# Two-layer network behind attention: the state-row softmax turned in 32x32 blocks by VectorE in place of TensorE's transposes, and the first batch's steps in another order

## The reference

```
scores  = scale * x @ state.T          # softmax over the 32 state rows   -> a
xread   = a @ state                    # 512 rows
scores2 = scale * state @ x.T          # softmax over the 512 positions   -> a2
sread   = a2 @ x                       # 32 rows
tokens  = concat([xread, sread], rows), heads side by side   # 4352 x 512
h = tokens @ w_in                      # 2048 wide
y = (h * clip(h + 3, 0, 6) / 6) @ w_out
```

## Time and profile before

| | us |
|---|---|
| median of 3 runs (1226.36 to 1226.95) | 1226.95 |
| the profiled execution | 1227.15 |
| its span | 1225.3 |
| TensorE busy | 1189.3 |
| VectorE busy | 580.4 |
| ScalarE busy | 445.3 |

### The profile page before, as it was taken

The page is one execution under the profiler, slowest core; times in us unless marked ns, Lnnn a source line. Parts: engine busy times, 40 slices in busy tenths (PEclk is TensorE's granted clock), DMA queues, the critical chain, the costliest instruction groups (busy, mean ns, idle before and its releaser), DMA issues.

```text
span 1225.3 us, 20849 instructions
## 1 busy us (share of the span) xinstructions
PE 1189.3 (97%) x6808; PEld 939.2 (77%) x6809; DVE 580.4 (47%) x1100; ACT 445.3 (36%) x741; POOL 84.0 (7%) x96
## 2 busy tenths in 40 slices
PE   7999999999999999999999978999999999999995
PEld 6777777777777777777778866888888888878874
DVE  4564645645547455465554373553532223455221
ACT  3454434443444344443544332341411112344110
POOL 0000100101001000010010110200000000000000
PEclk8999999999999999999999988999999999999998
DMA  9110100001001111010100662514151110541111
GB/s 369 63 36 1 69 36 35 36 35 70 35 14 56 36 47 58 1 70 1 69 36 1 221 207 100 179 43 175 37 179 52 34 51 28 181 163 44 41 36 42
DMA packets 32266, 91.45 MB, mean 75 GB/s; under 512 B 2879, under 2 KB 4031, under 8 KB 29632
## 3 DMA queue, kind: packets, MB, share of 16 engines
q1 hardware_dynamic: 26432, 72.56, 17.0%
q0 software_dynamic: 5760, 17.90, 3.8%
HBM read 65.95 MB, written 25.55 MB: 75 GB/s over the span
## 4 chain that ended last, share of the span: by engine, by line
PE 93%; DVE 3%; ACT 1%; issue 1%; DMA 0%; DVEq 0%; ACTq 0%; POOL 0%; SPq 0%; POOLq 0%
PE y_ps L829 30%; PE h_ps L894 17%; PE y_ps L920 17%; PE h_ps L814 14%; PE y_ps L906 3%; PE a_ps L789 2%; PE h_ps L804 2%; PE a_ps L876 1%; PE a_ps L679 1%; PE a_ps L767 1%; PE a_ps L740 1%; PE b_ps L687 1%; DVE we L462 1%; PE b_ps L679 0%; DMA x_t<-in_x_t 0%
## 5 line engine op out<-in xcount | busy, mean ns | idle before, releaser
L829 PE MATMUL y_ps<-w_out_hi,hid_hi 128*128 128x512 f32 x544 | 220.4, 405 | 0.3 <-DVE w_out_lo L1328 0.3
L829 PE MATMUL y_ps<-w_out_hi,hid_lo 128*128 128x512 f32 x544 | 212.8, 391 | 0.0
L829 PE MATMUL y_ps<-w_out_lo,hid_hi 128*128 128x512 f32 x544 | 212.5, 391 | 0.0
L894 PE MATMUL h_ps<-we,xg_t_hi 128*128 (+1 forms) x608 | 195.5, 403 | 4.6 <-DVE we L462 2.0
L920 PE MATMUL y_ps<-we,act_t_hi 128*128 (+1 forms) x608 | 191.4, 396 | 2.2 <-issue 2.2
L814 PE MATMUL h_ps<-att_hi,mix 128*128 128x512 f32 x512 | 186.6, 408 | 0.0
L1343 DVE SCALAR_TENSOR_TENSOR hid<-hid,h_ps 128x512 f32<-128x512 f32 (+1 forms) x144 | 94.4, 655 | 182.8 <-ACT hid L1038 181.3
L1038 ACT ACTIVATE hid<-h_ps,three 128x512 f32<-128x512 f32 (+1 forms) x144 | 95.5, 663 | 204.2 <-PE h_ps L814 180.8
L829 PEld LDWEIGHTS y_ps<-w_out_hi,hid_hi 128*128 128x128 f32 x544 | 102.1, 188 | 51.2 <-issue 30.4
L894 PEld LDWEIGHTS h_ps<-we,xg_t_hi 128*128 128x128 f32 x608 | 112.2, 189 | 30.6 <-issue 6.2
L920 PEld LDWEIGHTS y_ps<-we,act_t_hi 128*128 128x128 f32 x608 | 111.4, 188 | 24.3 <-issue 2.7
(11 more groups left out here) (227 smaller groups left out, 1341.6 us busy)
## 6 DMA issues: line engine op xcount, KB each, us to landing
raw<-in_w SPq DMA_DIRECT2D x14, 2048.0 KB, 8.8
xg<-buckets SPq DMA_DIRECT2D x41, 258.0 KB, 2.6
xb<-in_x_rows SPq DMA_DIRECT2D x8, 1024.0 KB, 4.8
x_t<-in_x_t SPq DMA_DIRECT2D x7, 1024.0 KB, 5.5
buckets<-pad_row SPq DMA_DIRECT2D x8, 774.0 KB, 8.6
w_in_raw<-in_w_in SPq DMA_DIRECT2D x4, 1024.0 KB, 13.2
raw_out<-in_w_out SPq DMA_DIRECT2D x4, 1024.0 KB, 14.8
x_t_second<-in_x_t SPq DMA_DIRECT2D x1, 1024.0 KB, 19.7
```

Source lines behind the costliest of these rows:

```text
L829: i = pe.matmul(y_ps[:, t, :], (hid_hi, hid_lo)[hp][:, hid_at(b, j), t * P:(t + 1) * P], w_out_s[wp][:, j, :], start=(j == 0 and m == 0), ...
L894: i = pe.matmul(hid_ps[:, h, :], xg_t[xp][:, slot % 2, k, :], we[:, bass.ds(w_at + (wp * WPART + k * F + h * BANK), BANK)], start=(k == 0 ...
```

## The change

Scores stay in their PSUM banks. VectorE's block transpose (`dve.transpose`) turns each 32x32 block of a 128x512 bank in its place and writes the result to `sc1` (step TURN): since the 32 state rows of a head lie in 32 partitions, each block then holds 32 positions in partitions and the 32 state rows along them. The softmax over state rows runs on `sc1` in this form, as 16 blocks of 32 per group, and one NORM1 per group. The same operation turns `sc1` back into `att1_raw` (step BACK), which lies on `att1_lo`; A1 then splits it with no TensorE step. The steps S2 and TensorE's part of A1, the copies to `sc_t` and the buffer `sc_t_first` are gone; SOFT2 reads the bank for both the maximum and the exponential. A bank that held scores is free once it is turned and its exponential is done. The tables are written anew: the opening does each group by itself and M(0) last, at half 7; in batch 0's block SOFT2 is at halves 0 and 2 and M(1) at half 4. `SPLIT_OUT` puts parts 2 and 3 at slices 8 and 11 (before 9 and 13). `WARM` is 75 products after half 0 and 92 after half 7 (before 45, 25 and 12).

```diff
@@ -117,9 +117,10 @@
...
     late_at = o
-    sc1 = at("sc1", o, [P, CH, H * NS], F32)
...
-    sc_t = at("sc_t", o, [P, GROUPS, S], F32)
...
+    BLOCKS = S // NS
+    sc1 = at("sc1", o, [P, GROUPS, BLOCKS, NS], F32)
     o += 4096
@@ -280,16 +281,17 @@
...
-    ATT = {14: [("S1", 0)], 15: [("SOFT2", 0)], 16: [("SOFT2", 1), ("S2", 0), ("MAX1", 0)],
-           17: [("S2", 1), ("MAX1", 1), ("DIF1", 0), ("DIF1", 1)], 18: [("NORM2", 0), ("EXP1", 0)],
-           19: [("NORM2", 1), ("EXP1", 1)], 21: [("NORM1", 0)], 22: [("A2", 0)], 23: [("A2", 1)], 25: [("SR", 0)],
-           27: [("SRT", 0)], 30: [("A1", 0)], 31: [("A1", 1)]}
...
-    ATT_FIRST = {0: [("S1", 0)], 1: [("S2", 0), ("MAX1", 0)], 2: [("S2", 1), ("MAX1", 1)],
-                 3: [("DIF1", 0), ("EXP1", 0), ("DIF1", 1), ("EXP1", 1)], 4: [("M", 0)], 5: [("NORM1", 0)],
-                 10: [("A1", 0)], 11: [("A1", 1)]}
...
-    ATT_REST = {0: [("M", 1)], 4: [("SOFT2", 0)], 5: [("SOFT2", 1)], 6: [("NORM2", 0)], 7: [("NORM2", 1)],
+    ATT = {14: [("S1", 0)], 15: [("TURN", 0), ("SOFT2", 0)], 16: [("TURN", 1), ("SOFT2", 1)],
+           17: [("MAX1", 0), ("MAX1", 1)], 18: [("DIF1", 0), ("EXP1", 0), ("DIF1", 1), ("EXP1", 1)],
+           19: [("NORM2", 0)], 21: [("NORM2", 1)], 22: [("A2", 0)], 23: [("A2", 1)],
+           24: [("NORM1", 0)], 25: [("SR", 0), ("NORM1", 1)], 27: [("SRT", 0)],
+           30: [("BACK", 0), ("BACK", 1)], 31: [("A1", 0), ("A1", 1)]}
...
+    ATT_FIRST = {0: [("S1", 0), ("TURN", 0), ("MAX1", 0)], 1: [("DIF1", 0), ("EXP1", 0)],
+                 2: [("TURN", 1), ("MAX1", 1)], 3: [("DIF1", 1), ("EXP1", 1)], 4: [("NORM1", 0), ("BACK", 0)],
+                 5: [("NORM1", 1), ("BACK", 1)], 6: [("A1", 0), ("A1", 1)], 7: [("M", 0)]}
...
+    ATT_REST = {0: [("SOFT2", 0)], 2: [("SOFT2", 1)], 4: [("M", 1), ("NORM2", 0)], 5: [("NORM2", 1)],
                 8: [("A2", 0)], 9: [("A2", 1)], 12: [("SR", 0)], 13: [("SRT", 0)]}
@@ -300,16 +302,16 @@
...
     BANK_OF |= {("T4", n): n % 2 for n in range(CH)} | {("L4", 0): 1, ("LT", 0): 0}
-    BANK_OF |= {(name, n): n for name in ("S2", "A2", "A1") for n in range(GROUPS)} | {("SR", 0): 0, ("SRT", 0): 0}
+    BANK_OF |= {(name, n): n for name in ("A2",) for n in range(GROUPS)} | {("SR", 0): 0, ("SRT", 0): 0}
...
     SPLIT_OUT_FIRST = 6
-    SPLIT_OUT = {5: 1, 9: 2, 13: 3}
+    SPLIT_OUT = {5: 1, 8: 2, 11: 3}
     SPLIT_IN = {3: 0, 6: 1, 9: 2, 13: 3}
...
-    WARM_START, WARM, WARM_ROWS = 60, {2: 45, 5: 25, 11: 12}, 100
+    WARM_START, WARM, WARM_ROWS = 60, {0: 75, 7: 92}, 100
@@ -347,16 +349,17 @@
...
         if not before_it:
-            return None if is_b(b, -1) else bank_free(b - 1, HALF, k)
+            return () if is_b(b, -1) else bank_free(b - 1, HALF, k)
         name, n, a = before_it[-1]
-        return {"T": ("rows_t_ready", CH * a + n + 1), "L": ("logits_ready", CH * a + n + 1),
+        if name == "S1":
+            return ("sc1_turned", GROUPS * a + k + 1), ("exp2_ready", GROUPS * a + k + 1)
+        return ({"T": ("rows_t_ready", CH * a + n + 1), "L": ("logits_ready", CH * a + n + 1),
                 "T4": ("rows_t_ready", CH * a + n + 1), "L4": ("logits_t_ready", a + 1),
...
                 "R": ("place_all", a + 1), "C": ("pad_base_ready", 1),
-                "S1": ("sc_t_ready0" if k == 0 else "sc_t_ready1", a + 1),
-                "S2": ("dif1_ready", GROUPS * a + n + 1), "A2": ("att2_t_ready", GROUPS * a + n + 1),
-                "SR": ("sr_rows_ready", a + 1), "SRT": ("sread_ready", a + 1), "A1": ("att1_t_ready", GROUPS * a + n + 1),
-                "M": ("mix_ready", GROUPS * (MIXES * a + n) + k + 1)}[name]
+                "A2": ("att2_t_ready", GROUPS * a + n + 1),
+                "SR": ("sr_rows_ready", a + 1), "SRT": ("sread_ready", a + 1),
+                "M": ("mix_ready", GROUPS * (MIXES * a + n) + k + 1)}[name],)
@@ -721,12 +721,12 @@
...
-                if k is not None and (free := bank_free(b, half, k)) is not None:
+                for free in bank_free(b, half, k) if k is not None else ():
                     wait(pe, *free)
@@ -740,17 +740,10 @@
...
                     i.then_inc(sem("s1_ps"), 1)
-                elif name == "S2":
+                elif name == "A2":
...
                         pe.wait_ge(sem("const_b"), 2)
-                    wait(pe, f"sc_t_ready{n}", a + 1)
-                    for c in range(CH):
-                        i = pe.transpose(bank_ap(k)[:, c * P:(c + 1) * P], scores_t(a)[:, n, c * P:(c + 1) * P],
-                                         ident[:])
-                    i.then_inc(sem("s2_ps"), 1)
-                elif name == "A2":
@@ -772,16 +765,10 @@
...
                     pe.transpose(bank_ap(k)[:, 0:P], sr_rows[:], ident[:]).then_inc(sem("srt_ps"), 1)
-                elif name == "A1":
...
-                    wait(pe, "att1_ready", a + 1)
-                    for c in range(CH):
-                        i = pe.transpose(bank_ap(k)[:, c * P:(c + 1) * P], sc1[:, c, n * P:(n + 1) * P], ident[:])
-                    i.then_inc(sem("a1_ps"), 1)
                 elif name == "M":
...
                     for g in range(GROUPS):
-                        if (name, n, a) != FIRST_MIX and (free := bank_free(b, half, g)) is not None:
+                        for free in bank_free(b, half, g) if (name, n, a) != FIRST_MIX else ():
                             wait(pe, *free)
@@ -981,18 +968,12 @@
...
                                        ).then_inc(sem("mix_hi"), 1)
-                elif name == "S1":
...
-                    wait(act, "s1_ps", a + 1)
...
-                    wait(act, "a1_ps", GROUPS * a)
-                    act.activation(scores_t(a)[:, 0, :], bank_ap(0), ACT.Copy).then_inc(sem("sc_t_ready0"), 1)
                 elif name == "SOFT2":
...
                     wait(act, "srt_ps", a)
-                    act.activation(att2[:, n, :], scores_t(a)[:, n, :], ACT.Exp, bias=nmax2[:, n:n + 1],
+                    act.activation(att2[:, n, :], bank_ap(n), ACT.Exp, bias=nmax2[:, n:n + 1],
                                    scale=SCALE, accum_out=sum2[:, n:n + 1]
@@ -1000,15 +981,11 @@
...
-                    wait(act, "h_ps", KF * a)
-                    wait(act, "a1_ps", GROUPS * a + n + 1)
-                    act.activation(att1_hi[:, n, :], bank_ap(k), ACT.Copy
-                                   ).then_inc(sem("att1_hi_ready"), 1)
+                    wait(act, "att1_back", GROUPS * a + n + 1)
+                    act.activation(att1_hi[:, n, :], att1_raw[:, n, :], ACT.Copy).then_inc(sem("att1_hi_ready"), 1)
                 elif name == "EXP1":
                     wait(act, "dif1_ready", GROUPS * a + n + 1)
-                    own = sc1[:, :, n * P:(n + 1) * P]
-                    act.activation(own, own, ACT.Exp, scale=SCALE).then_inc(sem("exp1_ready"), 1)
+                    act.activation(sc1[:, n], sc1[:, n], ACT.Exp, scale=SCALE).then_inc(sem("exp1_ready"), 1)
@@ -1022,9 +999,6 @@
...
                 act.wait_ge(sem("s1_ps"), 2)
-            elif c == 3:
-                act.wait_ge(sem("s2_ps"), GROUPS)
-                act.wait_ge(sem("exp2_ready"), GROUPS)
             act.activation(w_out_s[HI][:, GO * c:GO * c + GO, :], raw_out[:, GO * c:GO * c + GO, :], ACT.Copy
@@ -1185,13 +1158,13 @@
...
                                           ).then_inc(sem("mix_ready"), 1)
-                elif name == "S1":
+                elif name == "TURN":
                     wait(dve, "s1_ps", a + 1)
-                    wait(dve, "a1_ps", GROUPS * a)
-                    dve.tensor_copy(scores_t(a)[:, 1, :], bank_ap(1)).then_inc(sem("sc_t_ready1"), 1)
+                    wait(dve, "att1_back", GROUPS * (a - 1) + n + 1)
+                    dve.transpose(sc1[:, n].rearrange("p k m -> p (k m)"), bank_ap(n)).then_inc(sem("sc1_turned"), 1)
                 elif name == "SOFT2":
-                    wait(dve, f"sc_t_ready{n}", a + 1)
-                    dve.tensor_reduce(nmax2[:, n:n + 1], scores_t(a)[:, n, :], AX.X, ALU.max, negate=True
+                    wait(dve, "s1_ps", a + 1)
+                    dve.tensor_reduce(nmax2[:, n:n + 1], bank_ap(n), AX.X, ALU.max, negate=True
                                       ).then_inc(sem("nmax2_raw"), 1)
@@ -1205,16 +1178,21 @@
...
                                     ).then_inc(sem("sread_ready"), 1)
+                elif name == "BACK":
...
+                    wait(dve, "h_ps", KF * a)
+                    wait(dve, "att1_ready", GROUPS * a + n + 1)
+                    dve.transpose(att1_raw[:, n, :], sc1[:, n].rearrange("p k m -> p (k m)")
+                                  ).then_inc(sem("att1_back"), 1)
                 elif name == "A1":
...
                     wait(dve, "att1_hi_ready", GROUPS * a + n + 1)
-                    dve.tensor_tensor(att1_lo[:, n, :], bank_ap(k), att1_hi[:, n, :].bitcast(F32),
+                    dve.tensor_tensor(att1_lo[:, n, :], att1_raw[:, n, :], att1_hi[:, n, :].bitcast(F32),
```

(17 more changed lines are left out.)

23 lines of the change are left out of this document (10 added, 13 removed).

## The result

The changed kernel takes 1218.29 us (median of 4 runs, 1216.52 to 1219.24). The kernel before, on the same chip, takes 1226.65 (4 runs, 1225.58 to 1226.95). The ratio is 0.9932, interval 0.9915 to 0.9949. Forecast were 1219.0 and a range of 1215 to 1224. The profiled execution took 1218.93, its span is 1217.1 (before 1227.15 and 1225.3).

What follows compares the result with a forecast made beforehand. TensorE was taken as the bound, except in the first 29 us, where VectorE and ScalarE are. Transposes -12.3, opening +5.3, old stalls -2.3, new stalls +1.3 sum to -8.0: median 1219.0 us, range 1215 to 1224.

Steps and rivals of the forecast that it cites:

- 28 groups of transposes: Blocks of batches 0 to 6: S2's and A1's groups of four leave TensorE, 0.44 us each, 12.3 us off.
- first second-layer product late, at full clock: Opening: M(1,0) waits for both groups' exponentials, so this product starts at 31.4 for 28.55, 2.85 us later.
- half clock: Opening: after TensorE idles until 30.3, 3.4 to 6 us at half clock cost 1.7 to 3.0 us, taken as 2.5.
- stalls of before gone: Batch 0's block: earlier NORM2 and earlier w_out splits remove three TensorE stalls, 2.3 us off.
- new stalls in block 0: Batch 0's block: about 0.9 us at A2(0) and 0.4 at M(0,1), together +1.3 (0 to 2.5).
- part 4: Batch 0's block: three old stalls go, -2.3 us; new stalls at A2(0) and M(0,1) add 1.3.
- part 1: TensorE's transposes in the blocks: -12.3 us at 0.44 per group; durations in sequence would give 31 us.
- part 2: Blocks: VectorE gains about 2.8 us per batch, about 22 in all; steady blocks 1 to 6 pay nothing.
- (b): Block transpose on VectorE is dear, near 1.2 us; the opening lengthens, the run takes 1222; chance 0.11.
- (d): Slower than before through the opening's chain if a block transpose takes 2.35 us or more; 1231 at 3 us; chance 0.06.
- part 3: Opening: first product near 21.4, then M(1,0) held by the exponentials and clock loss; +5.3 us in all.
- rival (a): Opening nearly free: the clock holds over the gap before M(1), the run takes 1216.6; chance 0.14.

Runs made afterwards that it cites:

- experiment 1: Changed kernel plus two unread groups of four TensorE transposes in each block of batches 0 to 6: 1223.59 us, ratio 0.9971 to the kernel before.
- Experiment 2: Changed kernel with each TURN and BACK of batches 1 to 7 done twice by VectorE: 1221.32 us, ratio 0.9948 to the kernel before.
- Experiments 3: Changed kernel with M(1,0) written into two unused banks of y_ps and moved to half 2: 1214.62 us, ratio 0.9896 to the kernel before.
- 5: Kernel before the change with only M(1,0) moved from half 0 to half 4 of block 0: 1226.93 us against 1227.43, ratio 1.0.
- 8: Changed kernel with M(0) between A1's two parts, new WARM fillers and VectorE's split_out(0) after hid_lo(0): 1218.21 us, ratio 0.9923 to the kernel before.
- the repeat: The changed kernel run again unaltered, beside the kernel before: 1218.82 us, ratio 0.9934.
- experiment 6: Changed kernel with w_out's parts 2 and 3 split at slices 9 and 13 as before: 1223.4 us, ratio 0.9966 to the kernel before.

## Why the prediction was right, step by step

| step | predicted | measured |
|---|---|---|
| 28 groups of transposes | -12.3 | -10.6 in blocks 1 to 6; -1.76 put down for block 0, by the same price |
| first second-layer product late, at full clock | +2.85 | +2.5 |
| half clock | +2.5 | +1.55 |
| stalls of before gone | -2.3 | -2.3 |
| new stalls in block 0 | +1.3 | +1.65 |
| from the state tokens on | 0, 1 either way | +0.85 |
| sum | -8.0 | -8.1 by these rows, -8.2 in the spans |

The mechanism stands, with one exception (part 4). That the sum came out within 0.2 us is in part luck: the terms missed by -0.35, -0.95, +0.35 and +0.85 us, and these misses cancel.

**Transposes (part 1).** 0.44 us per group, read between starts, is what six blocks gave back to the hundredth (1.76 each), and experiment 1 priced it at 0.455 by adding such groups alone. The sequence price that part 1 weighed (31 us) is ruled out.

**VectorE (part 2).** A block transpose is 0.71 or 0.69 us, so rivals (b) and (d), at 1.2 and 2.35 us and more, are out. The groups that changed sum to 92.1 us for 72.9, +19; the forecast of 22 was made in the same way. The busy time of the page grew by 16.6 only. Over all of VectorE's groups the sum grew from 606.7 to 625.3, by 18.6; instructions overlap more in the kernel after, and the page counts an overlap once. At the end of a block the count of part 2 holds: in batch 1's, A1's second difference ends at 180.83, 4.9 us before the next block's first product, for the 4 of the prediction. Experiment 2 put another 2.8 us per block on VectorE and the steady blocks stayed as they were.

**The opening (part 3).** First product 21.4 predicted, 21.35 measured; M(1,0) released at 30.3, measured 29.99, by the instruction that was named (`exp2_ready`, the exponential at 28.95). Experiments 3, 5 and 8 show that this wait, and neither M's place nor the first product, sets the loss. Mis-sized is the half clock: 1.55 us, under the 1.7 of the prediction's lower bound. It lasted 3.4 us (30.4 to 33.8), the shorter of the two lengths in the prediction, and took 0.54 from M(1,0) and 1.01 from the second-layer products behind it. In the repeat the clock was lost in the other stretch, ahead of slice 0. So rival (a), the clock held over M(1,0)'s gap, does occur in executions of this very kernel, but with a loss elsewhere, and the medians are not 1216.6.

**Batch 0's block (part 4).** One stall at A2(0) near 77 us, as predicted (77.81), but by another cause. The rows in the timeline of the kernel after:

```profile
76.07 0.49 DVE L1204 TENSOR_SCALAR att<-att,sum 128x512 f32<-128x512 f32 x1
...
77.07 0.68 DVE L1157 TENSOR_TENSOR mix<-a_ps,mix 128x512 fp32r<-128x512 f32 x1
...
77.81 0.66 PE L749 MATMUL a_ps<-ident,att 128*128 128x128 f32 x4 [1.65 <-DVE mix L1157]
```

The prediction let A2(0) wait for NORM2 (`att2_ready`), 0.9 us. TensorE wanted A2(0) at 77.81 - 1.65 = 76.16 and `att` was ready at 76.56, so that wait would have been 0.4. What was later still was M(3)'s difference on VectorE, which frees the bank `a_ps` (77.07, ends at 77.75). The count missed that M(3), in the same bank, is served by the same full VectorE queue. The second new wait, 0.4 at M(0,1), did not come. The term was right to 0.35 us, its mechanism was not: that is luck. And the edit of SPLIT_OUT, counted as part of 2.3 us, is worth about 4.3 by the medians on top of the new order (experiment 6): with the old slices, DIF1 and EXP1 of batch 1 stand ahead of a split that TensorE needs. The sum didn't need that number, as both edits came together, but without it the rest of the change gains 4.0 us of 8.4.

**The rest.** From the state tokens to the end the spans vary from 565.9 to 569.1 between the profiled executions of all these kernels, which have the same program there. So the 0.85 is not put down to the change. Nor is a small loss ruled out: the two executions with the order of before took 566.4 and 566.6, the eleven others 567.8 in the mean.

Open: why the same program loses the clock in one idle stretch in one execution and in the other in the next. The traces show what goes with it (last section), but nothing was run that could settle the cause.

## What to carry to other kernels

Price an instruction on the bounding engine by what it adds between the starts of its neighbours in the stream, not by its duration. When a step keeps a buffer longer, look for the next user of that buffer and what stands behind it in its queue: here two banks held through an exponential cost about 4 us of a 12 us gain, and another pair of idle banks gave them back. Where an engine with spare time gets more work, check first the one stretch where its queue is already late, the first block here, rather than its average share.
